# Retention, gated FFN and routed FFN in one program: gate and value intermediates in PSUM, and another order of the splits and of the normalising

## The chip, the cores and the metric

The kernel runs on one core of one Trainium2 chip. The metric is the device time of one execution in microseconds (us). Before the change it is 885.03 us, the median of 3 runs (884.99 to 886.29).

## The reference

All inputs are fp32. Three stages follow each other:

```python
scores = (1/sqrt(64)) * q @ k^T            # 4 batches, 8 heads, 576 positions, 64 columns
ret = scores * Dmat                        # Dmat[i,j] = gamma_h ** (i-j) for i >= j, else 0
x = (ret @ v) as rows                      # 2304 tokens x 512

xn = x / sqrt(mean(x*x, -1) + 1e-6) * rms_g
g = xn @ w_gate;  val = xn @ w_val         # 512 -> 1536
x2 = (g * sigmoid(g) * val) @ w_out        # 1536 -> 512

e = argmax(x2 @ gate, 1)                   # one of 8 experts per token
out = softmax(..)[e] * sigmoid(x2 @ w_output_gate)[e] * (relu(x2 @ w1[e]) @ w2[e])
```

## The kernel before

Every fp32 product is made of three fp32r matmuls: each operand is split into a high part H (a ScalarE copy that rounds, `ACT.Copy` into fp32r) and a low part L (the value minus H, on GpSimd or VectorE), and TensorE adds H*H, H*L and L*H into one PSUM bank. So a tile that TensorE reads has passed two other engines in turn.

**Attention** (0 to about 98 us) runs over 16 units (4 batches x 4 pairs of heads). VectorE multiplies the scores by the decay mask, GpSimd scales the queries and adds squares, ScalarE evacuates the result into `xs`. Between the units' own instructions VectorE also computes 1/rms of finished batches (`root`: the three steps HALVE, TIMES, FIX, lines 694 to 698) and normalises (`normalise`, L706), by a table of unit numbers in `lag`.

**Gated FFN** (about 98 to 560 us) takes the tokens in three blocks of 768, in two halves of 384. A block has an up phase and a down phase, each over `f` = 0 to 11, 128 hidden columns at a time; `n` numbers all 36 of them.
- Up: gate and value products of both halves are one 2x2 block product, done with seven products m1 to m7 (a Strassen-Winograd scheme) of six matmuls of 384 columns: 42 matmuls (L1447 to L1449) an iteration. Its operands are sums of weights (`s_ab`, four of them, split into AH and AL) and sums of x (T1, T2, T3, NT4, made in place in `xs`, split into BH and BL once per block). The three results are put together on VectorE: `g0`, `g1` (L812, L823), `hv` = g times sigmoid (L826, L829), the value `v1` (L833) and `hid` (L836, L842). ScalarE copies partial sums (`p_y`, `p_m5`, `p_z`) and makes the two sigmoids (L1157).
- Down: per `f` two groups of nine matmuls of 512 columns (`down1(n, 0)` and `down1(n, 1)`, L1503 to L1505), one for each half of the tokens, into three banks each that collect over all `f`. A group needs hidH (ScalarE L1135), hidL (VectorE L849), dH (ScalarE L1128) and dL (GpSimd L521). hidH and hidL have one buffer per half: hidH of the next `f` waits until the group that read the last one has ended. dH and dL have two.

PSUM has 8 banks. X (banks 6 and 1), Y (0) and Z (7) hold the up products; the down groups collect in banks 0, 6, 2 and 3, 4, 5. In the up phase banks 2 to 5 hold only the last block's down results until ScalarE has taken them (`take_y`).

The order of the work on each engine is written out by hand: every engine has its own loop over the same `f`, with waits on semaphores. The last up iteration and the first down group are interleaved on TensorE: m6, down1(n0, 0), m7, down1(n0, 1), m4, down1(n0+1, 0), ... VectorE works between the products through lists of tasks: in block 0's up phase `IN_UP` (the roots of batch 2 and the normalising of eight pieces of 384 columns, one per iteration), in block 0's down phase `IN_DOWN` (the roots of batch 3 and eight more pieces), and in blocks 0 and 1 the sums T (`DOWN_T`) of the next block; ScalarE and GpSimd split the next block's x by `DOWN_B`.

ScalarE's order in a down step is the one that the change touches most:

```python
high_hidden(2 * (n + 1))        # hidH, half 0: waits for down1(n, 0)
high_down(n + 2)                # dH: waits for down1(n, 1)
high_hidden(2 * (n + 1) + 1)    # hidH, half 1: waits for down1(n, 1)
```

**Routing and routed FFN** (about 560 to 875 us) are not touched.

## Time and profile before

| | |
|---|---|
| median of 3 runs | 885.03 us |
| profiled execution: its own time | 877.32 us |
| its span | 875.5 us |
| TensorE busy / VectorE / ScalarE / GpSimd | 802.6 / 553.2 / 421.6 / 448.1 us |
| mean granted TensorE clock | 0.979 |
| the chain that ended last | PE 65%, DVE 11%, POOL 8%, issue 7%, ACT 4% |
| L1447 to L1449, up products | 1512 matmuls |
| L1503 to L1505, down groups | 648 matmuls |

PE is TensorE (PEld its weight loads), DVE VectorE, ACT ScalarE, POOL GpSimd. A row of a timeline gives start, length, engine, line, operation, what it writes and reads, and in brackets how long the engine had been idle and what released it. Matmuls overlap: the next one starts before the last has ended, so the time that one costs is the distance from start to start.

### The profile page before, as it was taken

What the parts mean: (1) busy time and instruction counts of PE and PEld (TensorE: products, weight loads), DVE (VectorE), ACT (ScalarE), POOL (GpSimd) and SP (SyncE); (2) the same over time, 40 slices, a digit from 0 to 9 for tenths busy, and PEclk for the clock granted to TensorE, in tenths of its full rate; (3) what the DMA queues carried; (4) which work ended last, traced back from release to release, by engine and by line L of the source; (5) the groups of instructions that cost most, each with busy time, mean ns of one, the idle gap of its engine ahead of it and who ended that gap; (6) DMA issues with size and microseconds to landing.
All of it is one profiled execution on the core that took longest, in us unless ns stands there. A gap on an engine that the chain in (4) does not pass through costs nothing.

```text
span 875.5 us, 14875 instructions
## 1 busy us (share of the span) xinstructions
PE 802.6 (92%) x5053; PEld 701.1 (80%) x5053; DVE 553.2 (63%) x804; ACT 421.6 (48%) x813; POOL 448.1 (51%) x378
## 2 busy tenths in 40 slices
PE   7989899988999999788999988978899999999995
PEld 6868788886679998566999966747688888888884
DVE  2589799997757888763788633353354555455453
ACT  3465655543436555343665423543355455455453
POOL 3478788886528889652888522147121121121121
PEclk9999999999999999999999999989999999999998
DMA  8982122122111242211124012306545555555553
GB/s 310 312 267 87 49 97 73 50 83 73 48 37 49 73 144 85 68 53 37 49 73 144 25 49 56 123 5 115 152 155 169 165 168 167 169 167 166 174 163 104
DMA packets 48362, 99.66 MB, mean 114 GB/s; under 512 B 7489, under 2 KB 8643, under 8 KB 48294
## 3 DMA queue, kind: packets, MB, share of 16 engines
q1 hardware_dynamic: 42934, 87.40, 32.1%
q0 software_dynamic: 4944, 10.96, 4.2%
q8 instruction: 31, 0.51, 0.2%
q10 hardware_dynamic: 432, 0.63, 0.2%
q14 instruction: 21, 0.17, 0.1%
HBM read 89.50 MB, written 10.40 MB: 114 GB/s over the span
## 4 chain that ended last, share of the span: by engine, by line
PE 65%; DVE 11%; POOL 8%; issue 7%; ACT 4%; DMA 2%; POOLq 0%; SPq 0%; ACTq 0%; DVEq 0%
PE banks L1447 7%; PE banks L1449 7%; PE banks L1448 7%; DVE hidL L849 5%; PE banks L1645 5%; PE banks L1646 5%; PE banks L1647 5%; PE banks L1503 4%; PE banks L1431 4%; PE banks L1432 4%; PE banks L1433 4%; PE banks L1505 3%; PE banks L1504 3%; POOL AL L509 3%; ACT hidH L1135 2%
## 5 line engine op out<-in xcount | busy, mean ns | idle before, releaser
L1447 PE MATMUL banks<-BH,AH 128*128 128x384 f32 x504 | 172.4, 342 | 12.3 <-DVE g L812 7.1
L1449 PE MATMUL banks<-BH,AL 128*128 128x384 f32 x504 | 169.4, 336 | 0.0
L1448 PE MATMUL banks<-BL,AH 128*128 128x384 f32 x504 | 169.2, 336 | 0.0
L849 DVE TENSOR_TENSOR hidL<-hid,hidH 128x384 fp32r<-128x384 f32 x72 | 76.6, 1065 | 65.4 <-ACT hidH L1135 65.4
L1447 PEld LDWEIGHTS banks<-BH,AH 128*128 128x128 f32 x504 | 95.2, 189 | 20.0 <-DVE g L812 10.3
L1503 PE MATMUL banks<-dH,hidH 128*128 128x512 f32 x216 | 89.4, 414 | 23.6 <-DVE hidL L849 23.3
L509 POOL TENSOR_TENSOR AL<-s_ab,AH 128x1024 fp32r<-128x1024 f32 x36 | 96.1, 2669 | 9.1 <-ACT AH L1113 8.4
L1448 PEld LDWEIGHTS banks<-BL,AH 128*128 128x128 f32 x504 | 95.3, 189 | 0.3
L1449 PEld LDWEIGHTS banks<-BH,AL 128*128 128x128 f32 x504 | 95.0, 189 | 0.0
L521 POOL TENSOR_TENSOR dL<-wraw,dH 128x512 fp32r<-128x512 f32 x36 | 47.0, 1304 | 87.4 <-ACT dH L1128 87.4
L1505 PE MATMUL banks<-dH,hidL 128*128 128x512 f32 x216 | 86.3, 399 | 0.0
L1504 PE MATMUL banks<-dL,hidH 128*128 128x512 f32 x216 | 86.1, 399 | 0.0
L1431 PE MATMUL banks<-xgH,wH 128*128 x256 | 82.2, 321 | 1.8 <-DVE xgL L979 1.0
L1432 PE MATMUL banks<-xgL,wH 128*128 x256 | 81.5, 318 | 0.0
L1433 PE MATMUL banks<-xgH,wL 128*128 x256 | 81.4, 318 | 0.0
L1503 PEld LDWEIGHTS banks<-dH,hidH 128*128 128x128 f32 x216 | 41.3, 191 | 47.4 <-POOL dL L521 25.5
L1645 PE MATMUL banks<-wH,h2H 128*112 128x512 f32 x192 | 77.5, 404 | 0.0
L1646 PE MATMUL banks<-wL,h2H 128*112 128x512 f32 x192 | 76.2, 397 | 0.0
L1647 PE MATMUL banks<-wH,h2L 128*112 128x512 f32 x192 | 75.8, 395 | 0.0
L984 DVE TENSOR_TENSOR wL<-wraw,wH 128x512 fp32r<-128x512 f32 x66 | 45.6, 693 | 47.6 <-ACT wH L1290 47.2
L635 POOL DMA_INDIRECT out<-yo,rec_cur x24 | 23.1, 961 | 96.8 <-ACT yo L1304 94.3
L1290 ACT ACTIVATE wH<-wraw 128x512 fp32r<-128x512 f32 x66 | 41.5, 630 | 47.4 <-DMA wraw<-w_moe 47.4
(190 smaller groups left out, 1718.2 us busy)
## 6 DMA issues: line engine op xcount, KB each, us to landing
wraw<-w_moe SPq DMA_DIRECT2D x168, 256.0 KB, 3.1
wraw<-w_moe SPq DMA_DIRECT2D x36, 512.0 KB, 3.6
vr<-v_rows SPq DMA_DIRECT2D x15, 320.0 KB, 4.9
qt<-q_t SPq DMA_DIRECT2D x16, 288.0 KB, 5.2
y_rows<-y_sb SPq DMA_DIRECT2D x6, 768.0 KB, 6.1
kt<-k_t SPq DMA_DIRECT2D x15, 288.0 KB, 4.2
kr<-k_rows SPq DMA_DIRECT2D x16, 256.0 KB, 3.4
mask<-c_mask SPq DMA_DIRECT2D x4, 160.0 KB, 5.4
```

The costliest lines, as they stand in the source:

```text
L509: nc.gpsimd.tensor_tensor(AL[:, n % 2, S1:S4 + 1, :], s_ab[:], AH[:, n % 2, S1:S4 + 1, :].bitcast(F32), ALU.subtract).then_inc(s_LS, 1)
L849: V.tensor_tensor(hidL[:, a, :], hid[:, n % F1, a * HALF:(a + 1) * HALF], hidH[:, a, :].bitcast(F32), ALU.subtract).then_inc(s_hidL, 1)
L1431: mm(out_ap, wh, xh, start=first, stop=False)
L1432: mm(out_ap, wh, xl, start=False, stop=False)
L1433: return mm(out_ap, wl, xh, start=False, stop=last)
L1447: mm(to, wh, bh, start=first and k == 0, stop=False, skip_group_check=True)
L1448: mm(to, wh, bl, start=False, stop=False, skip_group_check=True)
L1449: i = mm(to, wl, bh, start=False, stop=k == 1, skip_group_check=True)
L1503: mm(o, hidH[:, a, t], dH[:, p, :], start=f == 0, stop=False)
L1645: mm(o, h2H[:, p, t], wH[:, p, w], start=f == 0, stop=False)
L1646: mm(o, h2H[:, p, t], wL[:, p, w], start=False, stop=False)
L1647: mm(o, h2L[:, p, t], wH[:, p, w], start=False, stop=f == F2 - 1).then_inc(s_down2, 1)
```

## The change

It has five parts. (1) The two sigmoids go to PSUM banks 2 and 3 and the value sum to bank 5, in place of the SBUF tiles `sig` and `v1`. (2) In the down phase ScalarE makes both hidH before dH; the first hidden splits are moved some places ahead at the end of the up phase. (3) GpSimd's splits BL and dL, and VectorE's sums T, come in two instructions of half the size. (4) The normalising of the eight pieces of 384 columns leaves block 0's up phase for its down phase (with rows 2 and 3 of each piece first), and batch 3's large pieces leave block 0's down phase for block 1's; a copy of 1/rms of batch 1 (`late[:, 4]`, one ScalarE instruction) keeps it. (5) In the attention stage the weight sums of n = 0 and 1 are made at units 8 and 11, two on VectorE and two on GpSimd (before: all four on VectorE, at units 9 and 15).

```diff
         X, Y, Z = (6, 1), 0, 7
+        SIG, VAL, COPY = (2, 3), 5, (7, 1)
...
-        DOWN_B = {0: B21, 1: B11, 2: B22, 3: T1, 5: T2, 6: T3, 7: NT4}
+        DOWN_B = {1: B21, 2: B11, 3: B22, 6: T1, 7: T2, 8: T3, 9: NT4}
@@ gpsimd: low_b, low_down, units
-                nc.gpsimd.tensor_tensor(BL[:, b], src, BH[:, b].bitcast(F32), ALU.subtract).then_inc(s_BL, 1)
+                for k in range(2):
+                    i = nc.gpsimd.tensor_tensor(BL[:, b, k], src[:, k], BH[:, b, k].bitcast(F32), ALU.subtract)
+                i.then_inc(s_BL, 1)
...
-                    nc.gpsimd.tensor_tensor(dL[:, n % 2, :], wraw[:, n % 2, UPC:W1COLS], dH[:, n % 2, :].bitcast(F32),
-                                            ALU.subtract).then_inc(s_dL, 1)
+                    for h in range(2):
+                        c, w = slice(h * HK, (h + 1) * HK), slice(UPC + h * HK, UPC + (h + 1) * HK)
+                        i = nc.gpsimd.tensor_tensor(dL[:, n % 2, c], wraw[:, n % 2, w], dH[:, n % 2, c].bitcast(F32), ALU.subtract)
+                    i.then_inc(s_dL, 1)
...
+                if u == 8:
+                    sums_a(0)
+                    low_a(0)
@@ vector: hidden
-                V.tensor_tensor(hv[:, 0:1, :], g0[:], sig[:, 0:1, :], ALU.mult).then_inc(s_hv0, 1)
+                V.tensor_tensor(hv[:, 0:1, :], g0[:], banks[:, SIG[0]:SIG[0] + 1, 0:HALF], ALU.mult).then_inc(s_hv0, 1)
...
-                V.tensor_tensor(v1[:], x, p_m5[:], ALU.add).then_inc(s_v1, 1)
+                if n == 0:
+                    dve.wait_ge(s_sq, UNITS)
+                elif f == 0:
+                    dve.wait_ge(s_y, n // F1 * 2 * TPH)
+                wait(dve, s_h1, n)
+                val = banks[:, VAL:VAL + 1, 0:HALF]
+                V.tensor_tensor(val, x, p_m5[:], ALU.add).then_inc(s_v1, 1)
...
-                V.tensor_tensor(hid[:, f:f + 1, HALF:BLOCK], hv[:, 1:2, :], v1[:], ALU.mult).then_inc(s_h1, 1)
+                V.tensor_tensor(hid[:, f:f + 1, HALF:BLOCK], hv[:, 1:2, :], val, ALU.mult).then_inc(s_h1, 1)
@@ vector: tasks
-            IN_UP = [root_task(2, i) for i in range(3)] + [norm_task(q, k) for q in (2, 3) for k in range(KD)]
-            IN_DOWN = [root_task(3, i) for i in range(3)] + [norm_task(q, k) for q in (4, 5) for k in range(KD)]
-            DOWN_T = {0: T3, 1: T1, 4: T2, 6: NT4}
+            IN_UP = [root_task(2, i) for i in range(3)]
+            LATE_NORM = [root_task(3, i) for i in range(3)] + [norm_task(4, k) for k in range(KD)]
+            def down_tasks(blk):
+                parts = (2, 3) if blk == 1 else (5,)
+                tasks = [norm_task(q, k) for q in parts for k in ROWS_FIRST]
+                tasks += [lambda: None] * (2 * 4 - len(tasks))
+                tasks += [sum_task(blk, b, k) for b in (T3, T1, T2, NT4) for k in range(2)]
+                return tasks + (LATE_NORM if blk == 1 else [])
...
                 for f in range(F1):
-                    if f < F1 - 1:
+                    if 0 < f < F1 - 1:
                         low_hidden(2 * (n0 + f + 1))
+                    run(tasks[2 * f:2 * f + 1])
                     if f < F1 - 1:
                         low_hidden(2 * (n0 + f + 1) + 1)
+                    run(tasks[2 * f + 1:2 * f + 2])
@@ scalar: up_step, down_step
+                else:
+                    high_hidden(2 * (n - f + 1))
                 high_S(n + 2)
...
-                if blk > 0 and f < TPH:
-                    take_y(blk - 1, 1, f)
+                if n == 1:
+                    S.activation(late[:, 4, 0:SEQ], inverse(1), ACT.Copy).then_inc(s_keep, 1)
                 if f == F1 - 3:
                     high_down(n - f)
-                if f == F1 - 2:
                     high_hidden(2 * (n - f))
+                if f == F1 - 2:
                     high_hidden(2 * (n - f) + 1)
...
-                if f < F1 - 1:
+                if 0 < f < F1 - 1:
                     high_hidden(2 * (n + 1))
+                if f < F1 - 1:
+                    high_hidden(2 * (n + 1) + 1)
                 if f < F1 - 2:
                     high_down(n + 2)
-                if f < F1 - 1:
-                    high_hidden(2 * (n + 1) + 1)
@@ tensor: down1
+                    if f == 0 and DOWN[a][j] == SIG[0]:
+                        pe.wait_ge(s_hv0, n + F1)
+                    if f == 0 and DOWN[a][j] == VAL:
+                        pe.wait_ge(s_h1, n + F1)
```

The three `take_y` of the other half now stand at the head of the next block, around `copy_y(n0)` and `copy_m5(n0)`.

ScalarE's order in the first down steps of block 1, before:

```order
L1119 ACTIVATE AH<-wraw 128x256
L1135 ACTIVATE hidH<-hid 128x384
L1128 ACTIVATE dH<-wraw 128x512
L1135 ACTIVATE hidH<-hid 128x384
L1095 ACTIVATE BH<-xs 128x768
L1135 ACTIVATE hidH<-hid 128x384
L1128 ACTIVATE dH<-wraw 128x512
```

and now (x2 stands for two in a row):

```order
L1156 ACTIVATE hidH<-hid 128x384
L1149 ACTIVATE dH<-wraw 128x512
L1156 ACTIVATE hidH<-hid 128x384 x2
L1149 ACTIVATE dH<-wraw 128x512
L1118 ACTIVATE BH<-xs 128x768
```

dH has moved behind both hidH of a step, and BH comes one step later. VectorE's order from the last up iteration of block 0 on, before (first the iteration ahead of it, with its normalising L706):

```order
L836 TENSOR_TENSOR hid<-hv,v1 128x384
L706 SCALAR_TENSOR_TENSOR xs<-xs,gain_sb,late 128x384
L812 TENSOR_TENSOR g0<-banks,p_y 128x384
L842 TENSOR_TENSOR hid<-hv,banks 128x384
L849 TENSOR_TENSOR hidL<-hid,hidH 128x384
L742 TENSOR_TENSOR s_ab<-wraw 128x256
L743 TENSOR_TENSOR s_ab<-wraw 128x256
L823 TENSOR_TENSOR g1<-banks,p_z 128x384
```

and now, from `g1` of the last iteration into the down phase:

```order
L829 TENSOR_TENSOR g1<-banks,p_z 128x384
L832 TENSOR_TENSOR hv<-g0,banks 128x384
L835 TENSOR_TENSOR hv<-g1,banks 128x384
L861 TENSOR_TENSOR hidL<-hid,hidH 128x384
L845 TENSOR_TENSOR banks<-banks,p_m5 128x384
L848 TENSOR_TENSOR hid<-hv,banks 128x384
L861 TENSOR_TENSOR hidL<-hid,hidH 128x384
L854 TENSOR_TENSOR hid<-hv,banks 128x384
L720 SCALAR_TENSOR_TENSOR xs<-xs,gain_sb,late 128x384
L861 TENSOR_TENSOR hidL<-hid,hidH 128x384
```

The hidL that the second down step needs stands ahead of the last `hid` (L854), which waits for m4, and no normalising stands between the products any more; it follows in the down phase, between the hidL.

## Rows read from the trace of the kernel before

**Rows 1.** Waits over the span: us in total, times, longest us.

```profile
DVE hidL L849 <- ACT hidH L1135: 65.4, 55, 2.9
ACT dH L1128 <- PE banks L1505: 62.4, 28, 2.6
```

**Rows 2.** Timeline of PE, down steps of block 2: start us, us.

```profile
518.63 0.47 PE L1503 MATMUL banks<-dH,hidH 128*128 128x512 f32 x1 [0.62 <-DVE hidL L849]
...
522.36 0.39 PE L1504 MATMUL banks<-dL,hidH 128*128 128x512 f32 x1
522.59 0.39 PE L1505 MATMUL banks<-dH,hidL 128*128 128x512 f32 x1
523.59 0.47 PE L1503 MATMUL banks<-dH,hidH 128*128 128x512 f32 x1 [0.62 <-DVE hidL L849]
```

**Rows 3.** Timeline of ACT, DVE and POOL, the same step.

```profile
521.03 0.63 ACT L1128 ACTIVATE dH<-wraw 128x512 fp32r<-128x512 f32 x1 [2.40 <-PE banks L1505]
521.57 0.51 ACT L1135 ACTIVATE hidH<-hid 128x384 fp32r<-128x384 f32 x1
521.75 1.29 POOL L521 TENSOR_TENSOR dL<-wraw,dH 128x512 fp32r<-128x512 f32 x1 [3.67 <-ACT dH L1128]
522.11 1.33 DVE L849 TENSOR_TENSOR hidL<-hid,hidH 128x384 fp32r<-128x384 f32 x1 [2.89 <-ACT hidH L1135]
...
523.63 0.56 DVE L849 TENSOR_TENSOR hidL<-hid,hidH 128x384 fp32r<-128x384 f32 x1 [0.18 <-ACT hidH L1135]
```

**Rows 4.** Single lines: count, then min/median/max ns, first and last start.

```profile
L829 DVE TENSOR_TENSOR hv<-g,sig x36: 546/1084/1442, 103.4 to 500.0; 128x384 f32<-128x384 f32 x36
L836 DVE TENSOR_TENSOR hid<-hv,v x36: 557/1065/2164, 104.5 to 502.6; 128x384 f32<-128x384 f32 x36
L833 DVE TENSOR_TENSOR v<-banks,p_m x36: 544/546/560, 103.9 to 502.0; 128x384 f32<-128x384 f32 x36
L487 POOL TENSOR_TENSOR BL<-xs,BH x17: 1803/2156/2539, 61.9 to 395.1; 128x768 fp32r<-128x768 f32 x17
```

**Rows 5.** Busy us by stretch, all engines; then PEclk, DMA share, GB/s.

```profile
98.00:183.00 85.00, 78.84 (x432) 75.94 (x433) 77.21 (x101) 46.93 (x86) 71.31 (x53) 0.98 0.22 69
207.00:256.00 49.00, 44.64 (x181) 32.73 (x182) 35.62 (x34) 19.11 (x35) 24.36 (x15) 1.00 0.16 49
350.00:360.00 10.00, 6.51 (x23) 5.21 (x24) 8.77 (x7) 3.26 (x6) 8.00 (x5) 0.86 0.24 77
361.50:411.00 49.50, 44.39 (x185) 33.18 (x184) 28.66 (x23) 20.07 (x37) 24.30 (x15) 1.00 0.17 48
425.00:500.00 75.00, 75.00 (x429) 74.03 (x428) 60.15 (x91) 44.15 (x85) 62.03 (x47) 1.00 0.26 85
```

**Rows 6.** Busy us of L1447 alone, then of L1503 alone, 183 to 207 us.

```profile
183.00:207.00 24.00, 6.41 (x18) 3.51 (x18) 0.86 0.31 99
...
183.00:207.00 24.00, 4.81 (x10) 2.37 (x10) 0.86 0.31 99
```

**Rows 7.** Timeline of DVE and PE, one up iteration of block 0.

```profile
146.06 2.75 DVE L706 SCALAR_TENSOR_TENSOR xs<-xs,gain_sb,rinv 128x384 f32<-128x384 f32 x1
...
149.34 0.44 PE L1447 MATMUL banks<-BH,AH 128*128 128x384 f32 x1 [0.60 <-DVE g L812]
```

**Rows 8.** Timeline of PE where blocks 1 and 2 pass from up to down.

```profile
351.67 0.47 PE L1503 MATMUL banks<-dH,hidH 128*128 128x512 f32 x1 [2.06 <-DVE hidL L849]
...
357.62 0.63 PE L1505 MATMUL banks<-dH,hidL 128*128 128x512 f32 x1
...
506.69 0.48 PE L1503 MATMUL banks<-dH,hidH 128*128 128x512 f32 x1 [1.57 <-DVE hidL L849]
```

**Rows 9.** Timeline of DVE and PE, end of attention and first up products.

```profile
62.24 1.91 DVE L752 TENSOR_TENSOR s_ab<-wraw,s_ab 128x256 f32<-128x256 f32 x1
65.49 1.16 PE L1356 MATMUL banks<-qt,kt 64*128 64x128 f32 x16 [3.25 <-DVE probs L669]
...
97.96 0.69 PE L1447 MATMUL banks<-BH,AH 128*128 128x384 f32 x1 [2.83 <-ACT p_m L1146]
```

More of the change, by code:

```diff
@@ L1089, in high_b @@
                 if b in (B21, B11, B22):
[L1090 removed]
+                    act.wait_ge(s_xnf, NORMED[blk][b])
                 else:
[L1092 removed]
+                    act.wait_ge(s_T, 8 * blk + {T3: 2, T1: 4, T2: 6, NT4: 8}[b])
                 if b == B21:
@@ L1156, in gate @@
                 wait(act, s_hv1 if a else s_hv0, n)
-                S.activation(sig[:, a:a + 1, :], (g1 if a else g0)[:], ACT.Sigmoid).then_inc(s_sig1 if a else s_sig0, 1)
+                S.activation(banks[:, SIG[a]:SIG[a] + 1, 0:HALF], (g1 if a else g0)[:], ACT.Sigmoid).then_inc(s_sig1 if a else s_sig0, 1)
             def take_y(blk, a, j):
@@ L1171, in up_step @@
                     copy_y(n + 1)
+                else:
+                    high_hidden(2 * (n - f + 1))
                 high_S(n + 2)
@@ L1242, in _ @@
                 if blk > 0:
+                    take_y(blk - 1, 1, 0)
                     copy_y(n0)
+                    take_y(blk - 1, 1, 1)
                     copy_m5(n0)
+                    take_y(blk - 1, 1, 2)
                 for f in range(F1):
```

133 lines of the change are left out of this document (66 added, 67 removed).

## The prediction, on record before the change was run

> **What bounds the kernel now.** I read the waits first, then busy time by stretch, then single steps in the timeline. The waits name the pair that loses most: VectorE's hidL waits 65.4 us for ScalarE's hidH, and ScalarE's dH waits 62.4 us for TensorE's down groups [rows 1]. Stretches say where TensorE itself loses. In block 2's up phase it is busy 75.00 of 75 us with 429 matmuls, 0.175 us each [rows 5]; I take that as its pace for 384 columns. In block 0's up phase 432 matmuls took 85 us, against 432 x 0.175 = 75.6: 9.4 us lost, with VectorE busy 77.21 of 85. In the down phase one matmul follows the next after 0.23 us (522.36 to 522.59) [rows 2]. A step has 18, so 4.14 us, but steps start 4.96 us apart (518.63 to 523.59): 0.8 us lost in each. Of the stretches, 207 to 256 us lose 49 - 181 x 0.23 = 7.4, and 361.5 to 411 us lose 49.5 - 185 x 0.23 = 6.9 [rows 5]; block 2 has nine such gaps, 7.2. Together 21.5 us. The passage from up to down: 183 to 207 us hold 18 x 3 up matmuls and 10 x 3 down matmuls [rows 6], 9.5 + 6.9 = 16.4 us of work in 24: 7.6 us lost. Block 1's passage has gaps of the same kind, one of 2.06 us [rows 8], I count 7.6 again; block 2's lone gap is 1.57 us idle, some 1.8 with the lost overlap. Together 17 us.
>
> **Part 2 and 3, the down step.** After the second group of a step ScalarE first makes dH (521.03, hidH follows at 521.57), which lets GpSimd start dL at 521.75. hidL starts at 522.11 in dL's shadow and takes 1.33 us; alone it takes 0.56 [rows 3]. It ends at 523.44, TensorE goes on at 523.59, when it could have at 522.59 + 0.23 = 522.82. Its end lies 0.40 us behind dL's end (521.75 + 1.29 = 523.04), as if it had to wait for dL and then ran. With hidH first: hidH at 521.03 to 521.54, hidL 521.58 to 522.14, a matmul 0.15 later at 522.29. That is 0.5 us early, so the gap closes. dH then runs to 522.2, and dL to about 523.6, for a group that starts two groups later (above 524.8): 1.2 us to spare. Block 2, with nothing else in its down phase: 7.2 to about 0.5.
>
> Blocks 0 and 1 have BL and VectorE's tasks beside it. If instructions of GpSimd and two-operand SBUF instructions of VectorE exclude each other, block 0's down phase needs for GpSimd 12 dL x 1.29 + 7 BL x 2.15 = 30.5 us [rows 3, 4], and for VectorE 22 hidL, 8 normalising pieces, 8 half sums, at about 0.5 each, plus the three roots and four small pieces, about 3: 22. The halved instructions cost some 0.15 each more on GpSimd (an estimate: the head starts of rows 4, 2.16 - 1.80 = 0.36, halved and rounded down; nothing at the least, 0.36 at the most), 2.9 for 19. The sum, 55, is over the 12 x 4.14 = 49.7 us of TensorE. Against that, GpSimd prepares some of each instruction while it waits: the shortest BL is 1.80 us, the typical one 2.16 [rows 4]. I take a loss of 5 us for block 0 and, with four pieces in place of eight and no roots, 3 for block 1. Both ends: 0.5 if all interleaves well, 7 if the old loss stays. So 21.5 goes to 8.5: **13 us gained** (6.7 to 20).
>
> **Part 1, the PSUM banks.** hv L829 takes 546 at best and 1084 ns at the median, hid L836 557 and 1065, while L833, of the same 384 columns with one operand in PSUM, never leaves 544 to 560 [rows 4]. With sig and val in PSUM they (and L826, of the same form) should all take 0.55: 0.5 us off each of the two in each of 36 iterations, 1 us and a little for L826. It counts only where VectorE is late, in block 0. It also frees GpSimd; in blocks 1 and 2 TensorE has no gap to give back, and I count 1 us for both (0 to 2). No row shows a write of ScalarE or VectorE into PSUM: from below I take ScalarE's reads of PSUM and L833's 546 ns, from above the full double of it, 0.55 us more on v1, which delays m4 only if over 2 us. I take nothing.
>
> The Trainium skill (VectorE: DVE Perf Modes, the errata cycle table) speaks against it: a PSUM source costs VectorE 62 cycles of 0.96 GHz more than an SBUF one. By that the three instructions would be 0.2 us longer an iteration. The trace does not agree: 546 ns with a PSUM operand against 546 at best with two from SBUF.
>
> New waits: down1(n0, 0) waits for hv0 at its third bank, down1(n0, 1) for h1 at its third. hv0 is ready 1.2 us after m6, the third bank comes after 6 x 0.23 = 1.4. h1 is ready 1.3 us after m7 (two VectorE instructions), the bank again 1.4 later. Queued behind it are m4 and all down groups; it may cost 0.1 to 0.3 us a block. I count 0.3.
>
> **Part 4, normalising.** In block 0's up phase a piece of 384 columns takes 2.75 us on VectorE and g0 comes behind it, so TensorE stands 0.60 us, 0.77 with the overlap lost [rows 7]. Eight such go away. Three roots stay in the first iterations; two of them, contended, cost me 0.8 each. With part 1's 1 us beside it 9.4 goes to 1.6: **7.8 us gained** (6 to 9).
>
> **The passage.** The waits there come from hidH standing behind a split of ScalarE that waits for m4, and hidL behind that and behind normalising or T3. Now hidH of both halves is made one or two iterations earlier and hidL of the second step stands before the last hid. What is late next is hidL of the second step's other half: hidH behind AH, 1.1 us after m4, hidL 0.6 to 1.6 later with a normalising piece ahead of it, for a group that starts 2.07 after m4. That just fits. After such gaps the matmuls ran at 0.63 us in place of 0.39 [rows 8], the granted clock of 350 to 360 us being 0.86 [rows 5], so part of the time at the 1.2 GHz level; without the gaps I expect this gone. 17 goes to 2: **15 us gained** (9 to 16.5). If the clock still falls at each passage, it costs some 1.5 us a block.
>
> **Part 5, attention.** VectorE's two dependent weight sums leave it (1.91 us for the second) just ahead of the scores that TensorE waited 3.25 us for [rows 9]; at the end, four sums, a split of ScalarE behind them and then p_m5 gave a wait of 2.83. Against it: GpSimd, busy there too, takes four of the sums and waits for VectorE at units 8 and 11, with the query scaling of the next unit queued behind, and the split of T1 comes one unit later. Bounds 0 and 6.1 (both gaps). I take **4.5**. The `take_y` at the block heads, each about as long as a dH (0.63 [rows 3]), lie beside m2, m1, m5, 18 matmuls x 0.175 = 3.2 us; three of them are 1.9 and fit. The copy of 1/rms is another such instruction, on an engine busy 46.93 of 85 us [rows 5].
>
> **Sum.** 13 + 1 + 7.8 + 15 + 4.5 = 41.3, less 0.3: 41. On the profiled execution's own time, 877.3 (span 875.5), that is 836.3; the median of the runs lies 7.7 us higher, so 885.0 - 41 = **844 us**.
>
> **Rivals.**
> A. The port decides. GpSimd and VectorE exclude each other in the down phases of blocks 0 and 1, dL comes late and the old loss there stays: 6.7 in place of 13, and 35 in all, 850 us. For it: hidL's end at 0.40 behind dL's, and the sum of 55 against 49.7. Against: the halves let VectorE in sooner, and dL has 1.2 us to spare. The Trainium skill states the exclusion (SBUF — State Buffer, the shared port pair: a VectorE instruction with two SBUF inputs against a GpSimd one that reads SBUF, held for the whole instruction). Rows 3 agree; by that rule this rival is nearer.
> B. Everything runs at TensorE's pace, 0.5 lost per down phase and no clock fall: 20 + 2 + 9 + 16.5 + 4.5, 52 less, 833 us. For it: block 2's up phase does. Against: block 0's down phase has more work than time.
> C. GpSimd takes VectorE's place in attention: its queue waits for VectorE at units 8 and 11. 4.5 becomes 0 to -1: 849 us. For it: GpSimd gets four more instructions, and its waits are for the engine that is late there. Against: both gaps of rows 9 end with VectorE's sums, which leave.
> D. Slower: accesses to PSUM hold up TensorE's writes. Six new ones an iteration of 0.55 us, 3.3 us; if half of that stops TensorE, 1.65 x 36 = 59 more, 903 us. It decides from 1.15 us an iteration on (41 / 36). Against: in 425 to 500 us VectorE and ScalarE make seven reads of PSUM an iteration and TensorE is never idle [rows 5].
> E. The bank waits or hidH hold each passage as long as now: 15 becomes 0, 859 us.
>
> **Chances.** Forecast 0.45 (840 to 848), A 0.22, B 0.12, C 0.10, E 0.07, D 0.03, 0.01 for no change. The range 834 to 857 leaves out D, E and half of B. 0.2% (1.8 us) is what a measurement tells from no change; faster 0.96, same 0.01, slower 0.03.
>
> **What would show it.** Down steps of block 2 at 4.1 to 4.2 us, hidL there at 0.56; those of block 0 at 4.3 to 4.7. hv and hid at 0.55. Up iterations of block 0 at 7.3 us from the fourth on. A gap under 0.5 us at m4 of each passage, and no matmul of 0.63 us behind it. First m3 at 92 to 95 us in place of 97.96. A step of 4.9 in blocks 0 and 1 with waits for dL would speak for A. The forecast is wrong if the up iterations of blocks 1 and 2 get longer than 7.4 us.

## The result, and the profile after

The changed kernel takes 837.02 us (median of 4 runs, 836.85 to 838.86); beside it the kernel before took 885.01 (4 runs, 884.22 to 886.29). The ratio is 0.9461, with a 95% interval of 0.9444 to 0.9478: faster by 48.0 us, where 41 was forecast. The time lies in the range (834 to 857), 7 us under the forecast and below the likeliest case's own 840 to 848.

| | before | after |
|---|---|---|
| profiled execution / its span | 877.32 / 875.5 us | 838.86 / 837.2 us |
| TensorE busy | 802.6 us | 787.3 us (94%) |
| VectorE / ScalarE / GpSimd busy | 553.2 / 421.6 / 448.1 | 480.0 / 421.4 / 446.2 |
| granted clock | 0.979 | 0.982 |
| chain that ended last | PE 65%, DVE 11%, POOL 8%, issue 7% | PE 79%, POOL 7%, DVE 4%, issue 3% |

The medians differ by 48.0 us, the two profiled executions by 38.5 only: up to the last down matmul 47.3 are gained, and 8.8 of them are given back in the routed part, which no edit touches; the section on what was not expected shows where. So the parts are compared by landmarks in the timeline of TensorE, all ahead of the routed part. The table gives lengths in us. "Up" runs from the end of the last segment to m6 of the block's last up iteration (in block 0 from the first m3), "pass" from there to the first matmul of the third down step, "down" from there to the start of the last down matmul.

| | first m3 | up 0 | pass 0 | down 0 | up 1 | pass 1 | down 1 | up 2 | pass 2 | down 2 | last one at |
|---|---|---|---|---|---|---|---|---|---|---|---|
| before | 97.96 | 92.97 | 18.09 | 48.57 | 87.18 | 18.28 | 48.58 | 86.00 | 13.24 | 48.40 | 559.27 |
| after | 92.60 | 82.45 | 12.75 | 46.20 | 85.47 | 13.04 | 41.91 | 85.39 | 11.58 | 40.58 | 511.97 |
| gained | 5.4 | 10.5 | 5.3 | 2.4 | 1.7 | 5.2 | 6.7 | 0.6 | 1.7 | 7.8 | 47.3 |

Waits over the span, the answer to [rows 1] (us in total, times, longest):

```profile
ACT hidH L1156 <- PE banks L1538: 76.5, 61, 2.8
DVE hidL L861 <- ACT hidH L1156: 52.8, 42, 3.1
PE banks L1536 <- DVE hidL L861: 3.9, 8, 1.7
```

dH no longer waits for TensorE; hidH does. VectorE still waits 52.8 us for hidH, but that costs nothing now: what counts is that TensorE waits 3.9 us for hidL, eight times. TensorE's idle time before first matmuls (the page puts it at the H*H line) was 12.3 us for the up products and 23.6 for the down groups. The page's groups now (busy us, mean ns, then idle before):

```profile
L1474 PE MATMUL banks<-BH,AH 128*128 128x384 f32 x504 | 169.5, 336 | 2.5 <-ACT p_m L1167 1.7
...
L1536 PE MATMUL banks<-dH,hidH 128*128 128x512 f32 x216 | 86.1, 399 | 4.8 <-DVE hidL L861 3.9
```

One down step of block 2, the answer to [rows 2, 3]: ScalarE, VectorE, GpSimd, and, from the two steps ahead of it, two step starts of TensorE.

```profile
479.81 0.53 ACT L1156 ACTIVATE hidH<-hid 128x384 fp32r<-128x384 f32 x1 [1.51 <-PE banks L1538]
480.24 0.62 ACT L1149 ACTIVATE dH<-wraw 128x512 fp32r<-128x512 f32 x1
480.37 0.56 DVE L861 TENSOR_TENSOR hidL<-hid,hidH 128x384 fp32r<-128x384 f32 x1 [1.48 <-ACT hidH L1156]
480.94 1.43 POOL L528 TENSOR_TENSOR dL<-wraw,dH 128x256 fp32r<-128x256 f32 x2 [2.65 <-ACT dH L1149]
...
471.39 0.39 PE L1536 MATMUL banks<-dH,hidH 128*128 128x512 f32 x1
475.47 0.39 PE L1536 MATMUL banks<-dH,hidH 128*128 128x512 f32 x1
```

hidL starts at 480.37 and takes 0.56 us; dL, which waited for dH, starts at 480.94, when hidL is done. A step takes 4.08 us (471.39 to 475.47), and so do all nine in a row there; before it took 4.94 to 4.96.

Single lines, the answer to [rows 4] (min/median/max ns): the two gate products, the value sum into PSUM, hid, hidL, BL, dL, and the sigmoid.

```profile
L832 DVE TENSOR_TENSOR hv<-g,banks x36: 535/544/546, 96.6 to 461.5; 128x384 f32<-128x384 f32 x36
L835 DVE TENSOR_TENSOR hv<-g,banks x36: 553/555/556, 97.2 to 462.2; 128x384 f32<-128x384 f32 x36
L845 DVE TENSOR_TENSOR banks<-banks,p_m x36: 565/567/567, 98.1 to 464.2; 128x384 f32<-128x384 f32 x36
L848 DVE TENSOR_TENSOR hid<-hv,banks x36: 553/554/555, 98.7 to 464.8; 128x384 f32<-128x384 f32 x36
L861 DVE TENSOR_TENSOR hidL<-hid,hidH x72: 550/701/1374, 172.2 to 508.9; 128x384 fp32r<-128x384 f32 x72
L491 POOL TENSOR_TENSOR BL<-xs,BH x34: 991/1327/1721, 64.5 to 370.7; 128x384 fp32r<-128x384 f32 x34
L528 POOL TENSOR_TENSOR dL<-wraw,dH x72: 723/797/1253, 168.0 to 506.1; 128x256 fp32r<-128x256 f32 x72
L1178 ACT ACTIVATE banks<-g x72: 484/492/499, 94.3 to 461.6; 128x384 f32<-128x384 f32 x72
```

The four instructions of VectorE with an operand in PSUM stay at 535 to 567 ns in all 36 iterations; of the same form, hidL with all operands in SBUF still goes up to 1374.

Busy time by stretch, the answer to [rows 5]: up 0, down 0, down 1, up 2, down 2.

```profile
93.00:175.00 82.00, 81.28 (x468) 80.71 (x467) 58.37 (x103) 49.38 (x95) 69.51 (x58) 1.00 0.25 78
188.00:234.00 46.00, 42.66 (x180) 32.60 (x178) 37.09 (x40) 21.30 (x38) 35.33 (x32) 1.00 0.22 64
333.00:374.00 41.00, 40.99 (x177) 32.42 (x177) 23.20 (x29) 20.75 (x38) 32.31 (x32) 1.00 0.24 68
387.00:459.00 72.00, 72.00 (x417) 72.00 (x417) 49.11 (x89) 42.41 (x81) 55.33 (x49) 1.00 0.27 85
471.00:511.00 40.00, 40.00 (x178) 33.14 (x177) 10.61 (x19) 15.37 (x30) 12.90 (x18) 1.00 0.19 56
```

TensorE is idle for 3.3 of 46 us in block 0's down part and for 0.7 of 82 in its up phase; in the other three stretches it is busy throughout. The granted clock is 1.00 in all of them.

### The profile page after: what moved, and what is told of

Read it like the earlier page. It is cut to its first block, busy times and chain, and to the rows that moved or that the text cites. A ratio compares the mean times of both kernels' runs of the same rounds, so it can differ in the third digit from the quotient of the medians.

```text
span 837.2 us, 14959 instructions
## 1 busy us (share of the span) xinstructions
PE 787.3 (94%) x5053; PEld 696.7 (83%) x5053; DVE 480.0 (57%) x812; ACT 421.4 (50%) x814; POOL 446.2 (53%) x437
## 4 chain that ended last, share of the span: by engine, by line
PE 79%; POOL 7%; DVE 4%; issue 3%; ACT 2%; DMA 2%; another core or an unknown queue 2%; SPq 0%; POOLq 0%; ACTq 0%; DVEq 0%
PE banks L1474 9%; PE banks L1476 9%; PE banks L1475 9%; PE banks L1678 5%; PE banks L1679 5%; PE banks L1680 5%; PE banks L1536 5%; PE banks L1458 5%; PE banks L1459 5%; PE banks L1460 5%; PE banks L1538 4%; PE banks L1537 4%; POOL AL L514 2%; DVE hidL L861 2%
## 5 line engine op out<-in xcount | busy, mean ns | idle before, releaser
L1474 PE MATMUL banks<-BH,AH 128*128 128x384 f32 x504 | 169.5, 336 | 2.5 <-ACT p_m L1167 1.7
L514 POOL TENSOR_TENSOR AL<-s_ab,AH 128x1024 fp32r<-128x1024 f32 x36 | 89.5, 2486 | 20.6 <-ACT AH L1133 20.6
L1536 PE MATMUL banks<-dH,hidH 128*128 128x512 f32 x216 | 86.1, 399 | 4.8 <-DVE hidL L861 3.9
L528 POOL TENSOR_TENSOR dL<-wraw,dH 128x256 fp32r<-128x256 f32 x72 | 61.8, 879 | 53.0 <-ACT dH L1149 52.8
L861 DVE TENSOR_TENSOR hidL<-hid,hidH 128x384 fp32r<-128x384 f32 x72 | 58.4, 811 | 53.0 <-ACT hidH L1156 52.8
L1538 PE MATMUL banks<-dH,hidL 128*128 128x512 f32 x216 | 84.5, 391 | 0.0
L1537 PE MATMUL banks<-dL,hidH 128*128 128x512 f32 x216 | 84.3, 390 | 0.0
L1156 ACT ACTIVATE hidH<-hid 128x384 fp32r<-128x384 f32 x72 | 37.6, 523 | 76.5 <-PE banks L1538 76.5
L1007 DVE TENSOR_TENSOR wL<-wraw,wH 128x512 fp32r<-128x512 f32 x66 | 45.7, 693 | 35.5 <-ACT wH L1317 35.3
L1012 DVE TENSOR_TENSOR wL<-wraw,wH 128x512 fp32r<-128x512 f32 x65 | 44.8, 690 | 36.0 <-ACT wH L1324 32.5
```

What stands on the lines that cost most here:

```text
L1474: mm(to, wh, bh, start=first and k == 0, stop=False, skip_group_check=True)
L1536: mm(o, hidH[:, a, t], dH[:, p, :], start=f == 0, stop=False)
L1537: mm(o, hidH[:, a, t], dL[:, p, :], start=False, stop=False)
L1538: i = mm(o, hidL[:, a, t], dH[:, p, :], start=False, stop=f == F1 - 1)
```

## The experiments

All lengths are of the table's kind. Unless said otherwise an edit is to the changed kernel, and a length in brackets is the changed kernel's. The kernel before, profiled once more, shows how far two executions of one kernel lie apart here:

> The kernel before, unchanged, profiled once more. Its recorded profile took 877.3 us, its timed runs 885.0; the profiled time after the last down group was 316 us, in the changed kernel 325, where ScalarE stood 15.0 us at its first h2H although nothing there was changed. Theory: the routed part has an occasional or usual stall of ScalarE that the first profile of before missed and all else shows, so here the part after the last down group takes 323 to 325 us with a long wait of ScalarE at its first h2H, and the whole 884 to 886. Rival: the stall belongs to the changed kernel; then this profile shows 316 us again, and the 7.7 us of before lie elsewhere.

It took 886.96 us, 1 over the theory's range. The stall is there, 15.55 us, as the theory had it. Six of the nine segments from the first m3 on agree with the first execution within 0.2 us; pass 0 took 17.68 in place of 18.09, up 0 94.41 in place of 92.97, pass 1 19.86 in place of 18.28, and the last down matmul came at 561.86. The two large differences go with the granted clock: 0.53 in place of 0.76 over the 6.5 us behind the first m3, and 0.83 in place of 0.91 over pass 1. So a segment is good to some 0.3 us where the clock stays at 1.00, and to 1.6 where it fell; a difference of the whole time between two single executions of under 2 us says nothing. A part of the spread lies at the very start: a wait of TensorE in the attention stage that all kernels share ends between 54.74 and 57.20 us.

**1. dH between the two hidH again.**

```diff
-                if f < F1 - 1:
-                    high_hidden(2 * (n + 1) + 1)
                 if f < F1 - 2:
                     high_down(n + 2)
+                if f < F1 - 1:
+                    high_hidden(2 * (n + 1) + 1)
```

> The changed kernel with dH put back between the two hidH of each down step on ScalarE; all else as changed. Theory (the place of dH sets the step): block 2's down phase from its third step on goes from 40.6 back to 48.4 us, block 1's from 41.9 to about 48.5, block 0's from 46.2 to 49 to 51; in all 17 to 20 us more. Rival (halving GpSimd's pieces alone frees hidL from waiting, the place of dH does not matter): block 2 stays under 42.5 and the whole is less than 3 us longer.

846.50 us; down 48.29, 45.10, 43.40 (46.20, 41.91, 40.58). Neither expectation: of the 7.8 us that block 2 gained, 2.8 return; from the first m3 on the kernel is 8.2 us slower, between the rival's 3 and the theory's 17.

```profile
494.12 0.63 ACT L1149 ACTIVATE dH<-wraw 128x512 fp32r<-128x512 f32 x1 [1.82 <-PE banks L1538]
494.66 0.51 ACT L1156 ACTIVATE hidH<-hid 128x384 fp32r<-128x384 f32 x1
494.83 0.74 POOL L528 TENSOR_TENSOR dL<-wraw,dH 128x256 fp32r<-128x256 f32 x1 [2.65 <-ACT dH L1149]
495.20 0.78 DVE L861 TENSOR_TENSOR hidL<-hid,hidH 128x384 fp32r<-128x384 f32 x1 [2.31 <-ACT hidH L1156]
```

hidL starts inside dL again, but the half of dL ends at 495.57, and hidL at 495.98. It takes 0.78 us in place of 1.33 [rows 3]: it waits for the half that runs, not for the whole.

**2. Whole pieces.** BL and dL in one instruction each.

```diff
-                    for h in range(2):
-                        ...
-                        i = nc.gpsimd.tensor_tensor(dL[:, n % 2, c], wraw[:, n % 2, w], dH[:, n % 2, c].bitcast(F32), ALU.subtract)
-                    i.then_inc(s_dL, 1)
+                    nc.gpsimd.tensor_tensor(dL[:, n % 2, :], wraw[:, n % 2, UPC:W1COLS], dH[:, n % 2, :].bitcast(F32),
+                                            ALU.subtract).then_inc(s_dL, 1)
```

> The changed kernel with GpSimd's two splits BL (768 columns) and dL (512) made whole again, as before; ScalarE still makes both hidH ahead of dH. Lengths in the changed kernel's trace, from the third down step to the end of the last group: block 0 46.2, block 1 41.9, block 2 40.6 us; in the kernel before 48.6, 48.6, 48.4. Theory (order first): with hidH ahead of dH, hidL is made before GpSimd starts dL, so the size of dL is worth nothing in block 2 (40.6 to 41.0), and in blocks 0 and 1 the halves of BL are worth 1 to 4 us each. Last down group at 513 to 518 us (changed: 511.97). Rival (halving does it): the down steps of block 2 stand at 4.4 us or more, 43.5 or more for the block, and blocks 0 and 1 return to 46 to 48.6; last down group at 520 or later.

845.33 us; down 47.22, 44.83, 40.58; the passages 0.2 to 0.3 longer; the last down matmul at 516.82. In block 2 the halves are worth nothing once the order is right, in blocks 0 and 1 they are worth 1.0 and 2.9, in all 4.9 from the first m3 on: as the theory had it. Block 1, GpSimd, VectorE and TensorE:

```profile
363.16 2.13 POOL L490 TENSOR_TENSOR BL<-xs,BH 128x768 fp32r<-128x768 f32 x1
363.54 2.65 DVE L857 TENSOR_TENSOR hidL<-hid,hidH 128x384 fp32r<-128x384 f32 x2
365.86 0.47 PE L1532 MATMUL banks<-dH,hidH 128*128 128x512 f32 x1 [1.35 <-DVE hidL L857]
```

The first of the two hidL comes 0.4 us behind the start of a whole BL, takes 2.18 us and ends at 365.72, 0.43 behind BL's end (365.29); TensorE waits for it.

**3. The order alone, in the kernel before.** Nothing else of the change.

```diff
-                if f < F1 - 2:
-                    high_down(n + 2)
                 if f < F1 - 1:
                     high_hidden(2 * (n + 1) + 1)
+                if f < F1 - 2:
+                    high_down(n + 2)
```

> The kernel before with one edit: in a down step ScalarE makes both hidH before dH (nothing else of the change). Theory (order first): block 2's down part falls from 48.4 to 41 us or less, and blocks 0 and 1 from 48.6 to 43 to 46 each, since whole BL and VectorE's tasks still lie beside it; 11 to 18 us in all. Rival (the order needs the halves): less than 3 us in each block.

874.28 us beside 884.78, 10.5 less. Down 46.33, 45.63, 40.57, where before had 48.57, 48.58, 48.40: 13.0 us, within the theory's 11 to 18, though block 0 just misses its 43 to 46. Passes 0 to 2 took 16.75, 19.40 and 15.26, where before had 18.09, 18.28 and 13.24. That the order makes passes longer is not shown by this: the second execution of before needed 19.86 for pass 1, and in pass 2 TensorE's wait grew by 0.4 only (1.98 us, before 1.57), while the granted clock was 0.89 in place of 1.00 (table under edit 7).

**4. Gates and value sum in SBUF.**

```diff
-                S.activation(banks[:, SIG[a]:SIG[a] + 1, 0:HALF], (g1 if a else g0)[:], ACT.Sigmoid)...
+                S.activation(sig[:, a:a + 1, :], (g1 if a else g0)[:], ACT.Sigmoid)...
...
-                val = banks[:, VAL:VAL + 1, 0:HALF]
+                val = v1[:]
```

> The changed kernel with the sigmoids and the value sum in SBUF tiles as before; normalising stays in the down phase. Theory (in the up phase it is the normalising ahead of g0 that made TensorE wait, the banks matter little): hv and hid take 0.75 to 1.1 us again, the up iterations of blocks 1 and 2 go from 7.28 to 7.38 us, block 0's with them, in all 2 to 4 us more. Rival (VectorE's time was the limit in block 0, so the banks gave the larger share of the 10.5 us gained there): block 0's up phase 6 us or more longer.

843.41 us. Up 0 86.74 (82.45), up 1 86.62 (85.47), up 2 86.00 (85.39), passes 14.54, 14.77, 11.56 (12.75, 13.04, 11.58); down 0 43.97 (46.20). Block 0's up phase grew by 4.3 us, more than the theory's share and less than the rival's 6; from the first m3 on the whole is 6.9 longer. hv and hid take 833 to 1086 ns at the median again. The largest gaps stand behind block 0's three iterations with the roots, and inside the down group between m6 and m7, at its third bank:

```profile
102.41 0.45 PE L1476 MATMUL banks<-BH,AH 128*128 128x384 f32 x1 [1.17 <-DVE g L820]
110.79 0.44 PE L1476 MATMUL banks<-BH,AH 128*128 128x384 f32 x1 [0.79 <-DVE g L820]
182.35 0.50 PE L1538 MATMUL banks<-dH,hidH 128*128 128x512 f32 x1 [1.37 <-DVE hv L834]
```

The last one is TensorE's wait for hv0 before it writes the bank of the first sigmoid. The edit left that wait in, though nothing lies in the bank here; it costs 1.54 us in pass 0 and 1.53 in pass 1, where the changed kernel loses 0.63 and 0.61. So up to 1.8 of the 3.5 us by which the passages grew belong to that wait and not to the banks.

**5. The eight normalising pieces back in block 0's up phase**, gates in PSUM.

```diff
-            IN_UP = [root_task(2, i) for i in range(3)]
+            IN_UP = [root_task(2, i) for i in range(3)] + [norm_task(q, k) for q in (2, 3) for k in ROWS_FIRST]
...
-                parts = (2, 3) if blk == 1 else (5,)
+                parts = () if blk == 1 else (5,)
...
+                    if blk == 0 and f == F1 - 1:
+                        run(IN_UP[F1 - 2:F1 - 1])
```

> The changed kernel with the eight normalising pieces of 384 columns back in block 0's up phase (one each in iterations 3 to 9 and one in the last, ahead of g0 as before), gates in PSUM. Theory: a piece still waits for GpSimd's long split and makes g0 late, by 0.4 us where it was 0.77, so 3 us more in block 0's up phase; block 0's down phase has less port work and goes from 46.2 to 42 to 43.5, so the whole is within 1.5 us of the changed kernel. Rival A (the port does not set block 0's down phase): it stays at 45 or more and the whole is 3 us or more longer. Rival B (the up phase hides the pieces now that VectorE is faster): up phase unchanged, whole 3 to 4 us shorter.

837.81 us; up 0 82.70 (82.45), down 0 44.89 (46.20). The up phase is as rival B had it, the whole is 1.0 shorter where B had 3 to 4. With the gates in PSUM, moving the pieces out of the up phase was worth nothing: they hide there, and in the down part they cost 1.3.

**6. Edits 4 and 5 together.**

> The changed kernel with two parts undone together: gates and value sum in SBUF, and the eight normalising pieces (in the new order of pieces) back in block 0's up phase. Length from m3 of iteration 0 to m6 of the last, in block 0: before 92.97 us, changed 82.45, gates alone undone 86.74, normalising alone undone 82.70. Theory (either of the two parts suffices from the fourth iteration on, since an SBUF product behind a GpSimd instruction and a normalising piece only together make g0 late): 91 to 93.5 us, 4 or more beyond the gates alone. Rival (the banks alone cure the up phase, and what before lost besides came from whole BL): 88 or less.

Up 0 took 93.51 us, as before the change and at the edge of the theory's range. This run, edit 7 and the two better versions ran on another chip (see under 10 and 11), so of them lengths of segments are compared. The four corners:

| up 0, us | pieces in the up phase | pieces in the down phase |
|---|---|---|
| gates in SBUF | 93.51 | 86.74 |
| gates in PSUM | 82.70 | 82.45 |

The rows show why. One normalising piece with the gates in SBUF (this run; GpSimd's AL of the iteration, then VectorE), and one with them in PSUM (edit 5):

```profile
148.61 2.58 POOL L516 TENSOR_TENSOR AL<-s_ab,AH 128x1024 fp32r<-128x1024 f32 x1
148.86 2.75 DVE L722 SCALAR_TENSOR_TENSOR xs<-xs,gain_sb,late 128x384 f32<-128x384 f32 x1
```

```profile
143.18 0.61 DVE L720 SCALAR_TENSOR_TENSOR xs<-xs,gain_sb,late 128x384 f32<-128x384 f32 x1
143.31 2.74 POOL L514 TENSOR_TENSOR AL<-s_ab,AH 128x1024 fp32r<-128x1024 f32 x1 [0.34 <-ACT AH L1135]
```

The same instruction takes 2.75 us where it starts 0.25 us behind AL, and 0.61 where it starts 0.13 ahead of it. With the gates in SBUF the products ahead of it are slower (hv 0.88 us, which uses up the engine's idle 0.40, then hid 0.94, in place of 0.55 each), so it comes second, is done only when AL is, and g0 behind it is late: TensorE stands 0.6 us in each iteration with a piece.

**7. The splits of the passage as before.** hidH of the first down step both at the eleventh iteration, hidH and hidL of the second step in the down loop.

```diff
-                else:
-                    high_hidden(2 * (n - f + 1))
...
-                if 0 < f < F1 - 1:
+                if f < F1 - 1:
                     high_hidden(2 * (n + 1))
...
```

> The changed kernel with the hidden splits of the passage from up to down where they stood before: hidH of both halves at the eleventh up iteration, hidH and hidL of the second down step in the down loop, behind m4 and the last hid. The three passages (m6 of the last iteration to the third down step) take 12.75, 13.04, 11.58 us in the changed kernel; 18.09, 18.28, 13.24 before; 14.54, 14.63 in blocks 0 and 1 with the gates in SBUF. Theory (the order of the splits carries most of the passage): blocks 0 and 1 at 15.5 to 17.5 each, block 2 at 12.5 to 13.5, total 7 to 11 us over the changed kernel. Rival (the banks and the normalising that moved away carry it, the order is worth under 1 us each): blocks 0 and 1 at 13.8 or less, block 2 at 12.2 or less.

Passes 16.13, 14.45, 13.23 (12.75, 13.04, 11.58); down 0 43.97, down 1 41.48 (46.20, 41.91). In each passage one gap at the third down group:

```profile
184.85 0.47 PE L1533 MATMUL banks<-dH,hidH 128*128 128x512 f32 x1 [1.86 <-DVE hidL L861]
```

The three passages lose 6.4, but down 0 and down 1 give 2.7 back: from the first m3 on the kernel is only 3.7 us slower. Pass 1 missed the theory's bound by 1 us, and the whole missed its 7 to 11. Passes 0 and 1 differ by 1.7 with nearly the same gap (1.86 and 1.82), and the clock goes with it. Length in us and granted clock of each passage:

| | pass 0 | pass 1 | pass 2 |
|---|---|---|---|
| before | 18.09, 0.81 | 18.28, 0.91 | 13.24, 1.00 |
| before, second execution | 17.68, 1.00 | 19.86, 0.83 | 13.27, 1.00 |
| order alone (edit 3) | 16.75, 1.00 | 19.40, 0.82 | 15.26, 0.89 |
| splits as before (edit 7) | 16.13, 0.89 | 14.45, 1.00 | 13.23, 1.00 |
| after | 12.75, 1.00 | 13.04, 1.00 | 11.58, 1.00 |

Where the clock is at its 1.2 GHz level, the down matmuls follow each other after 0.43 us in place of 0.23 (edit 3, from 501.07 us on). All falls but the first of before's pass 0 begin within 0.8 us of the end of a wait of TensorE for hidL of 1.8 to 2.1 us. The same wait does not always bring one: it stands in pass 0 of before's second execution and in pass 1 of edit 7 (1.81 and 1.82 us), with the clock at 1.00. So some 1.7 us of the 6.4 are a fall of the clock in this one execution.

**8. The attention stage as before.**

```diff
-                if u == 8:
+                if u == 9:
                     sums_two(0)
-                if u == 11:
-                    sums_two(1)
+                    sums_rest(0)
...
+                    sums_two(1)
+                    sums_rest(1)
...
```

> The changed kernel with the weight sums of n = 0 and 1 and their splits where they were in the attention stage (four sums on VectorE, at units 9 and 15). Theory: the 5.4 us that the first m3 comes earlier (92.60 in place of 97.96 us) are all this part's: m3 at 97.5 to 98.5, everything behind it moved by the same, last down group at 517 to 518 us. Rival: the first m3 was late through T1 and the last normalising instead, and half or more of the 5.4 us stays: m3 at 95 or earlier.

The first m3 comes at 96.39 us in place of 92.60, with the gap for p_m back (2.87 us, before 2.83 [rows 9]) and one of 2.43 for the scores (before 3.25); the rest of the segments are unchanged but for up 0 (82.94). The theory had 97.5 or later. A part of the difference to before's 97.96 was there before the change begins to act, so the stretch from the shared early wait (56.04 us here) to the first m3 is the better measure. It takes 41.26 and 41.16 us in the two executions of before, 35.92 to 35.96 in the nine profiles with the new stage and halves, and 40.35 here: of 5.3 us, 4.4 are this part's. With whole pieces (edit 2) it takes 37.84, with the granted clock at 0.61 from 79 to 87 us: the halves are worth 1.9 here too.

```profile
96.39 0.69 PE L1479 MATMUL banks<-BH,AH 128*128 128x384 f32 x1 [2.87 <-ACT p_m L1173]
```

**9. The down weights first on SyncE's queue.**

```diff
                 for f in range(F1):
+                    if f >= F1 - 2:
+                        weights1_down(n0 + f - F1 + 4)
                     weights1_up(n0 + f + 4)
-                    if f >= F1 - 2:
-                        weights1_down(n0 + f - F1 + 4)
```

> The changed kernel with one edit on SyncE's queue: in the last two up iterations the weights of the down step are fetched ahead of those of the next up iteration. In the changed kernel ScalarE's dH at 191.04 us waits 2.45 us for a DMA and TensorE then stands 1.82 us at 193.72; block 1's passage has a dH that waits 0.90 us. Theory: the transfer issued too late is the cause, so the 1.82 gap is gone and block 0's down part falls from 46.2 to 44.0 to 44.8; the total by 1.5 to 2. Rival (the port decides: hidL there is late through GpSimd and VectorE): dH comes early and the gap stays within 0.5 us.

836.67 us; down 0 43.99 (46.20), without the gap of 1.66 us, as the theory had it; down 1 41.40 (41.91), the last down matmul at 509.73. The rows of the changed kernel, of SyncE's queue (L390 an up fetch, L395 a down fetch), ScalarE and TensorE, and then of this one:

```profile
185.14 0.33 SPq L390 DMA_DIRECT2D wraw<-w_moe  x1
185.51 8.01 SPq L395 DMA_DIRECT2D wraw<-w_moe  x3
...
191.04 0.63 ACT L1149 ACTIVATE dH<-wraw 128x512 fp32r<-128x512 f32 x1 [2.45 <-DMA wraw<-w_moe]
192.31 0.92 ACT L1156 ACTIVATE hidH<-hid 128x384 fp32r<-128x384 f32 x2
193.72 0.47 PE L1536 MATMUL banks<-dH,hidH 128*128 128x512 f32 x1 [1.66 <-DVE hidL L861]
```

```profile
178.25 0.33 SPq L395 DMA_DIRECT2D wraw<-w_moe  x1
...
189.00 0.62 ACT L1149 ACTIVATE dH<-wraw 128x512 fp32r<-128x512 f32 x1
```

With the shorter passage dH is wanted before its weights have arrived: their fetch (185.51) stood behind one of an up step (185.14), which waits for a buffer; put ahead of it, it goes out at 178.25. ScalarE stands 2.45 us, and hidH and hidL of the next group queue behind. TensorE's gap names hidL; the cause is a DMA two engines back. It also explains why edits 4 and 7, which make the passage longer, gave 2.2 back in down 0: their dH there (188.71 and 184.18 us) waits for no DMA, and TensorE has no such gap.

**10 and 11. Two better versions**, timed five and six times. The first has edit 9 and m5 ahead of m1 at the head of blocks 1 and 2; the second has besides all normalising and roots in the up phases. The edit to the heads:

```diff
+                if blk == 0:
                     m1(n0)
                     m5(n0)
+                else:
+                    m5(n0)
+                    m1(n0)
...
```

> The changed kernel with the down weights first on SyncE's queue (as in the run before), and m5 ahead of m1 at the head of blocks 1 and 2, since the first m3 of each block waits 0.58 us for ScalarE's copy of m5. Theory: 2 us from the weights and 0.6 to 0.75 from each of two block heads: 833.5 to 834.5 in place of 837.0. Rival (the copy of m1 is then late instead): nothing at the heads, 835.

> The run before this one (weights and m5 first), and all normalising and roots of batches 2 and 3 in the up phases (eight pieces in block 0's, the rest with batch 3's roots in block 1's), none in the down phases. With the gates in PSUM a piece in an up iteration cost nothing in block 0 (+0.3 us for eight). Theory: block 0's down part at 42.0 to 43.0 (44.0 with the weights alone), block 1's up phase unchanged but for up to 0.6, one more us gained in all: 832 to 834. Rival (VectorE is too full in block 1's up phase with its 3 roots and eight pieces, or GpSimd's BL of the down phase waits the longer for VectorE): 835 or more.

They ran on another chip, on which the kernel before took 876.55 us (873.78 to 881.07, 11 runs). The changed kernel was not timed there, so its ratio beside the 885 us is the measure: 824.7 us and 0.9406 (0.9378 to 0.9433) for the first, 823.8 and 0.9386 (0.9356 to 0.9416) for the second, against 0.9461 (0.9444 to 0.9478) for the change. Both intervals lie below the change's, as far as ratios carry over from chip to chip; by ratio the two can't be told apart. By segments: up 1 and up 2 84.60 and 84.54 (85.47, 85.39), down 0 43.98 in the first and 41.84 in the second, which takes 0.7 longer in up 1 and 0.4 in down 1. From the first m3 to the last down matmul they take 414.92 and 414.06 us, the changed kernel 419.37: 4.4 us from the weights and the heads (3.2 to 3.5 expected), and 0.9 from the normalising (1 expected). These lengths of single profiles, good to some 0.3 us a segment where the clock is 1.00, are the stronger evidence.

## Why the prediction was right

The sign, the mechanisms of four of the five parts (all but the normalising) and the range held. On the landmarks the forecast was 41 and 47.3 were gained. Term by term:

| term | predicted | measured |
|---|---|---|
| down steps | 13 (losses left 5, 3, 0.5) | 2.4 + 6.7 + 7.8 = 16.9 |
| passages | 15 | 5.3 + 5.2 + 1.7 = 12.2 |
| block 0's up phase | 7.8, with a share of the banks | 10.5 |
| up phases of blocks 1 and 2 | 1 | 2.3 |
| attention | 4.5 | 5.4 (4.4 by edit 8) |
| bank waits | -0.3 | -1.2, counted in the passages |

**Down steps.** The mechanism was right: hidH first brings hidL ahead of dL (hidL at 0.56 us, the step at 4.08; forecast 4.1 to 4.2). Edit 3 shows it alone: 7.8 us in block 2. What is mis-sized is the loss at both ends. Before, it was read as 21.5 us with 0.23 us a matmul; at block 2's present pace (40.58 us) it was 23.8. After, it was what the shared port leaves in the other blocks. 3 was set down for block 1; 41.91 against block 2's 40.58 is 1.3. Block 0 lost 5.6, near the 5 set down, but for another reason in part: 2.2 of it go with edit 9, and are a DMA, not the port. The sum of 55 us against 49.7 was too dark: by it the block could not have kept a step of 4.6 us on average, as it did. It took VectorE and GpSimd as never at work together; whether that is the reason no run isolates.

**Rival A** (the old loss stays where BL lies beside) was wrong in size and right in mechanism. With whole pieces 1.0 and 2.9 us come back (edit 2). In block 1 the three gaps that make up the 2.9 (0.79, 1.35 and 0.80 us) are each a hidL that stands behind a BL that started first; in block 0 so are three of six, the others stand behind a dL, a normalising piece or a root. The halves are what kept A small. The Trainium skill (SBUF — State Buffer, Who interferes with whom) says that issue order decides who blocks, for the whole instruction. The traces agree: hidL takes 1.33 us behind a whole dL [rows 3], 0.78 behind half of one (edit 1), and a piece takes 2.75 or 0.61 by a start 0.25 behind AL or 0.13 ahead (edits 6 and 5).

**The banks and the normalising.** Here the sum was too low (7.8 for 10.5) and its attribution wrong. Most of the 7.8 us were the eight pieces, at 0.77 each; PSUM stood beside them as 1 us less of VectorE's time an iteration, without a share of its own. The four corners turn this round: with the gates in PSUM the move is worth 0.3 in the up phase and costs 1.3 in the down part, while PSUM is worth 10.8 with the pieces in place and 4.3 without them. What failed is the step by which a piece "takes 2.75 us on VectorE" in this phase. That is not the piece's time; it is its time when it starts behind AL, and PSUM changed which came first. It was luck that this did not hurt the number: the change makes both edits, and either one takes most of the loss away. Of the 1.6 left for the roots only one gap came, 0.72 us idle at m7 of iteration 0 (0.88 with the overlap lost).

The ScalarE side was unpriced. The Trainium skill (ScalarE: Activation LUTs, Step-by-step: what each stage is for) calls PSUM the faster destination. The sigmoid took 492 ns into PSUM and 525 into SBUF, so the trace agrees: 33 ns each. The 62 cycles more for VectorE's PSUM source, which the prediction cites from the Trainium skill (VectorE: DVE Perf Modes, the errata cycle table) and sets aside, don't show after either: 544 to 567 ns at the median, where two SBUF operands take 546 at best [rows 4].

**The passages** were forecast at a gain of 15 from a loss of 17. By the landmarks the loss was 18.09 + 18.28 + 13.24 less three times 11.35 (18 x 0.1735 + 36 x 0.2285) = 15.6, and 3.3 is left. So 1.4 of the shortfall is the loss counted too high (7.6 for each of blocks 0 and 1, which was 6.7 and 6.9), and 1.3 is that 3.3 was left in place of 2. The bank waits are most of that: 0.63 and 0.61 us in blocks 0 and 1 where 0.3 in all was set down. The step that was wrong there is that hv0 is ready 1.2 us after m6:

```profile
175.91 1.80 POOL L528 TENSOR_TENSOR dL<-wraw,dH 128x256 fp32r<-128x256 f32 x2
176.15 0.96 DVE L757 TENSOR_TENSOR s_ab<-wraw 128x256 f32<-128x256 f32 x1
177.03 0.55 DVE L829 TENSOR_TENSOR g<-banks,p_z 128x384 f32<-128x384 f32 x1
177.50 0.54 DVE L832 TENSOR_TENSOR hv<-g,banks 128x384 f32<-128x384 f32 x1
178.10 0.50 PE L1536 MATMUL banks<-dH,hidH 128*128 128x512 f32 x1 [0.46 <-DVE hv L832]
```

m6 ends at 176.24, but VectorE is held until 177.1 by a weight sum that started behind dL and takes 0.96 us (0.41 at the median), and hv0 is ready at 178.04, 1.8 us after m6. "What is late next is hidL" was right as to the instruction, but the longest gap behind the passage, 1.66 us idle (1.82 with the overlap lost), came from dH's weights, which the prediction did not follow through SyncE's queue. By edit 7 the order of the splits is worth 6.4 us, 1.7 of them a fall of the clock; by edit 4 the banks are worth 3.5, 1.8 of them at a wait that the edit left in. The matmuls of 0.63 us behind a gap [rows 8] are gone, and the granted clock is 1.00 from 20 to 530 us, as forecast; before, it was 0.81 over pass 0 and 0.91 over pass 1, so a part of the 12.2 us gained is the clock, up to 1.6 a fall by the two executions of before.

**Attention** went as forecast and rival C did not come: TensorE now waits for GpSimd's query scaling three times, 1.8 us in all, in place of 3.25 for the scores and 2.83 for p_m [rows 9]. Rival D (PSUM accesses stall TensorE) is refuted: 72.00 of 72 us busy in up 2, and every iteration there takes 7.28 us where it took 7.28 to 7.41. The time came nearer to B (all at TensorE's pace, 833 us) than to the forecast: from it block 0's down part and the passages keep the kernel, 5.6 and 3.3 us.

The parts undone one at a time, from the first m3 on, are worth 8.2 (order), 4.9 (halves), 6.9 (banks), 3.7 (splits of the passage) and -1.2 (normalising), with 4.4 (weight sums) and 1.9 (halves) ahead of it: 29 in all, where 47.3 were gained. The rest is shared: parts that cure the same wait each look cheap while the other stays.

## What to carry to other kernels

Where two engines exclude each other, an instruction's time in a trace depends on who came first: before pricing a moved instruction by its row, look at what ran 0.2 us ahead of it. Get the critical operand's producer in front, cut the rival's instructions in half, and keep operands in PSUM where banks are free. When two edits cure the same wait, measure all four corners; undoing one at a time gave 4.3 and 0.3 us here, and both together 11.1. And look at the granted clock of a segment before giving its time to an edit: a fall was worth up to 1.7 us of a passage. When a stage gets shorter, follow the next operand back to its DMA's place in the queue: the gap will name another engine.
